# A fused linear-attention, capacity-routed expert and feed-forward kernel: the first search in pieces, and the first expert's second weights behind its rows

## What is computed

```python
# 1. gated linear attention: batch 4, 8 heads, 768 steps, head width 40
for t in range(S):
    m_new = max(f_gate + m, i_gate)
    C = exp(f_gate + m - m_new) * C + exp(i_gate - m_new) * outer(v, k)
    n = ... the same with k alone
    y[t] = sigmoid(o_gate) * (C @ q) / max(|n @ q|, 1)
x = y as 3072 rows of 320
# 2. routing: each token gets one of 8 experts, each expert 384 tokens
logits = x @ w_gate
for idx in argsort(-logits.flatten()):          # highest score first
    tok, e = idx // 8, idx % 8
    if not assigned[tok] and counts[e] < 384: assign tok to e
# 3. each expert
out[mask] = relu(x[mask] @ w1[e]) @ w2[e]       # 320 -> 1024 -> 320
# 4. on all rows
h = out @ w_in                                  # 320 -> 2048
result = (max(h, 0) + alpha * min(h, 0)) @ w_out
```

## Time and profile before

| | us |
|---|---|
| median of 3 runs | 823.14 (821.55 to 823.72) |
| the profiled execution | 826.35 |
| its span on the core | 824.6 |
| TensorE busy (share of the span) | 767.3 (93%) |
| VectorE busy | 585.4 (71%) |
| ScalarE busy | 323.3 (39%) |
| GpSimd busy | 166.5 (20%) |
| mean granted TensorE clock | 0.953 |

### The profile page before, as it was taken

The page is one execution under the profiler, slowest core; times in us unless marked ns, Lnnn a source line. Parts: engine busy times, 40 slices in busy tenths (PEclk is TensorE's granted clock), DMA queues, the critical chain, the costliest instruction groups (busy, mean ns, idle before and its releaser), DMA issues.

```text
span 824.6 us, 17035 instructions
## 1 busy us (share of the span) xinstructions
PE 767.3 (93%) x5535; PEld 719.1 (87%) x5535; DVE 585.4 (71%) x1454; ACT 323.3 (39%) x775; POOL 166.5 (20%) x244
## 2 busy tenths in 40 slices
PE   4999999984299999999999999999999999999995
PEld 3999999973188998899899889989998998999995
DVE  5766777766767886887787778768867886884442
ACT  4655666620213441452345135323613441352331
POOL 7356777510100011021001101100110110011001
PEclk9989999975589999999999999999999999999998
DMA  7787888510500410140041005003100400230000
GB/s 162 194 227 202 235 219 220 141 39 2 169 1 1 141 29 25 33 138 24 0 140 29 24 0 169 24 0 115 54 24 0 149 27 16 67 101 25 1 1 24
DMA packets 73407, 65.78 MB, mean 80 GB/s; under 512 B 35232, under 2 KB 64544, under 8 KB 73376
## 3 DMA queue, kind: packets, MB, share of 16 engines
q1 hardware_dynamic: 63584, 51.94, 22.7%
q0 software_dynamic: 2688, 8.65, 3.3%
q10 hardware_dynamic: 7104, 4.79, 1.8%
HBM read 56.71 MB, written 8.65 MB: 79 GB/s over the span
## 4 chain that ended last, share of the span: by engine, by line
PE 87%; DVE 8%; issue 2%; DMA 1%; ACT 1%; SPq 0%; POOL 0%; ACTq 0%; DVEq 0%
PE bank L825 19%; PE bank L827 17%; PE bank L826 17%; PE bank L668 6%; PE bank L715 5%; PE bank L843 4%; PE bank L844 4%; PE bank L703 2%; PE bank L696 2%; PE bank L679 2%; PE bank L749 1%; PE bank L660 1%; PE bank L868 1%; PE bank L869 1%; DMA s<-w 1%
## 5 line engine op out<-in xcount | busy, mean ns | idle before, releaser
L825 PE MATMUL bank<-wo_hi,h_hi 128*128 128x320 f32 x384 | 120.8, 315 | 0.0
L827 PE MATMUL bank<-wo_hi,h_lo 128*128 128x320 f32 x384 | 118.7, 309 | 0.0
L826 PE MATMUL bank<-wo_lo,h_hi 128*128 128x320 f32 x384 | 118.0, 307 | 0.0
L1484 DVE SCALAR_TENSOR_TENSOR g_act<-g_neg,rest_alpha,bank 128x384 f32<-128x384 f32 x128 | 78.6, 614 | 44.5 <-ACT g_neg L1058 43.5
L592 POOL DMA_INDIRECT xe<-x_rows,idx_in x24 | 24.4, 1015 | 407.0 <-DVE idx_in L1424 355.5
L1058 ACT ACTIVATE g_neg<-bank 128x384 f32<-128x384 f32 x128 | 62.8, 491 | 101.6 <-PE bank L844 101.6
L1056 ACT ACTIVATE h_hi<-bank 128x384 fp32r<-128x384 f32 x64 | 31.5, 491 | 170.4 <-PE bank L844 170.4
L1062 ACT CAST h_hi<-g_act 128x384 fp32r<-128x384 f32 x128 | 65.6, 512 | 79.5 <-DVE g_act L1484 79.0
L825 PE MATMUL bank<-yT_hi,wi_hi 128*128 128x384 f32 x256 | 92.3, 361 | 0.3 <-DVE yT_lo L1510 0.3
L827 PE MATMUL bank<-yT_hi,wi_lo 128*128 128x384 f32 x256 | 86.7, 339 | 0.0
L826 PE MATMUL bank<-yT_lo,wi_hi 128*128 128x384 f32 x256 | 86.7, 339 | 0.0
(11 more groups left out here) (229 smaller groups left out, 1834.2 us busy)
## 6 DMA issues: line engine op xcount, KB each, us to landing
s<-w SPq DMA_DIRECT2D x8, 1280.0 KB, 9.3
s<-w SPq DMA_DIRECT2D x8, 1024.0 KB, 5.2
s<-w SPq DMA_DIRECT2D x16, 256.0 KB, 6.2
k_in<-kT SPq DMA_DIRECT2D x24, 160.0 KB
q_wide<-qT SPq DMA_DIRECT2D x48, 80.0 KB
k_row<-k SPq DMA_DIRECT2D x24, 160.0 KB, 3.3
v_in<-v SPq DMA_DIRECT2D x24, 160.0 KB, 3.8
gate_o<-o SPq DMA_DIRECT2D x24, 160.0 KB, 3.0
```

What stands on the lines that cost most here:

```text
L825: pe.matmul(acc, ah, bh, start=start, stop=False, skip_group_check=True)
L826: pe.matmul(acc, ah, bl, start=False, stop=False, skip_group_check=True)
L827: return pe.matmul(acc, al, bh, start=False, stop=stop, skip_group_check=True)
L1484: dve.scalar_tensor_tensor(out=g_act[:, n, :], in0=g_neg[:, :], scalar=rest_alpha[:, j:j + 1], in1=acc, op0=ALU.mult, op1=ALU.add).then_in ...
```

## The change

- **Search.** `first_compare` works in three pieces of 10, 8 and 6 tiles (in the first step 20 and 4). The piece of 20 tiles is compared in `early_keys`, and `first_count` counts each piece as it comes; TensorE waits for the last logit's copy ahead of its first matmul. `first_flag` makes `flag` in one instruction with an accumulated output. Key values are scaled by 2^23, so that `keys_at_value` is one instruction.
- **Order of small steps.** In `make_keys` the maximum is taken and compared earlier, and three instructions are marked without a wait. The update of `route_value` goes from `take` to `reopen`; `closed_id` goes behind `member_sum`.
- **Rows.** `match_rows` makes each tile's one-hot rows with a `tensor_scalar` of 128 elements; `place_row` is now f32. This holds in all phases.
- **Weights.** In `load_weights` SP waits for `first_rows[1]` before it issues the first expert's second weights. ScalarE and VectorE take the rows before the second weights, whose last two thirds come behind `activate(0, 0)` and `split_hidden(0, 0)`.

Left out of the diff: `TOP`, `at_value` and `over_value` go, and `place_row` loses its BF16.

```diff
@@ -52,7 +52,8 @@
     assert REST == 64 and HB == 32 and CAP == 384 and S == NCH * P
-    VALUE_STEPS = [(5, 19), (5, 14), (5, 9), (5, 4), (4, 0)]
+    VALUE_AT = 23
+    VALUE_STEPS = [(5, VALUE_AT + 19), (5, VALUE_AT + 14), (5, VALUE_AT + 9), (5, VALUE_AT + 4), (4, VALUE_AT)]
     TIE_STEPS = [(5, 18), (5, 13), (5, 8), (5, 3)]
     STEPS = VALUE_STEPS + TIE_STEPS
     NS = len(STEPS)
...
@@ -352,6 +350,15 @@
             return slice(HB * (c % 4), HB * (c % 4) + HB)
+        def first_pieces(n):
+
+            ends = [0, NT - B, NT] if n == 0 else [0, 10, 18, NT]
+            return [slice(*pair) for pair in zip(ends, ends[1:])]
+
+        def pieces_before(n):
+
+            return sum(len(first_pieces(i)) for i in range(n))
+
         def bc(ap, n):
             return ap.unsqueeze(len(ap.shape)).to_broadcast(list(ap.shape) + [n])
@@ -455,6 +462,8 @@
                 sp.dma_start(s1[:, 0:2, :], w1[w, 0:2 * P, :].rearrange("(t p) f -> p t f", p=P)).then_inc(stage1_in, 16)
                 sp.dma_start(s1[0:REST, 2, :], w1[w, 2 * P:DM, :]).then_inc(stage1_in, 16)
                 sp.dma_start(s1[REST:P, 2, :], w1[w, 2 * P:DM, :]).then_inc(stage1_in, 16)
+                if first(e, 1):
+                    sp.wait_ge(first_rows[1], 16)
                 sp.dma_start(s2[:, :, :], w2[w].rearrange("(j p) d -> p j d", p=P)).then_inc(stage2_in, 16)
             load_weights(0)
@@ -752,9 +761,9 @@
             def first_count(n):
-                for half in range(2):
-                    pe.wait_ge(halves_ready, 2 * n + half + 1)
-                    for c in range(NT // 2 * half, NT // 2 * half + NT // 2):
+                for i, cs in enumerate(first_pieces(n)):
+                    pe.wait_ge(halves_ready, pieces_before(n) + i + 1)
+                    for c in range(cs.start, cs.stop):
                         ins = pe.matmul(CNT[0:JM, 0:E], above[:, JM * c:JM * c + JM], choice[:, c, :],
                                         start=(c == 0), stop=(c == NT - 1), skip_group_check=True)
                 ins.then_inc(count_ready, 1)
@@ -793,6 +802,7 @@
             pe.sem_inc(four_ready, NS)
+            pe.wait_ge(logit_read, NT)
             for n in range(NS):
                 first_count(n)
                 raise_base(0, n)
@@ -1041,8 +1051,6 @@
             for t in range(3):
                 high_w1(0, t)
-            for t in range(3):
-                high_w2(0, t)
             def rows_hi(e, t):
                 act.wait_ge(xe_turned, 3 * e + t + 1)
@@ -1083,7 +1091,10 @@
             for t in range(3):
                 rows_hi(0, t)
+            high_w2(0, 0)
             activate(0, 0)
+            high_w2(0, 1)
+            high_w2(0, 2)
             with act.Fori(0, E - 1) as e:
                 expert(e, True)
             expert(E - 1, False)
@@ -1169,12 +1180,15 @@
                 bits = logits[:, ts, :].bitcast(I32)
                 ch.link(dve.tensor_scalar(isign[:, ts, :], bits, 31, -2 ** 31, ALU.arith_shift_right, ALU.bitwise_or))
                 ch.link(dve.tensor_tensor(ibits[:, ts, :], bits, isign[:, ts, :], ALU.bitwise_xor))
-                ch.link(dve.tensor_scalar(isign[:, ts, :], ibits[:, ts, :], 8, None, ALU.logical_shift_right))
-                ch.mark(dve.tensor_copy(route_value[:, ts, :], isign[:, ts, :]))
+                ch.mark(dve.tensor_scalar(isign[:, ts, :], ibits[:, ts, :], 8, None, ALU.logical_shift_right))
                 ch.link(dve.tensor_scalar(ibits[:, ts, :], ibits[:, ts, :], 255, None, ALU.bitwise_and))
+                ch.mark(dve.tensor_scalar(route_value[:, ts, :], isign[:, ts, :], float(2 ** VALUE_AT), None, ALU.mult))
                 ch.link(dve.tensor_copy(tmp_a[:, ts, :], ibits[:, ts, :]))
+                ch.mark(dve.tensor_reduce(best_value[:, ts], route_value[:, ts, :], X, ALU.max))
                 ch.link(dve.scalar_tensor_tensor(out=route_tie[:, ts, :], in0=tmp_a[:, ts, :], scalar=float(2 ** 15), in1=route_tie[:, ts, :],
                                                  op0=ALU.mult, op1=ALU.add))
+                ch.link(dve.tensor_tensor(tmp_a[:, ts, :], route_value[:, ts, :], bc(best_value[:, ts], E), ALU.is_equal))
+                choose_tie(ch, ts)
             def choose_value(ch, ts):
@@ -1193,6 +1207,22 @@
                 choose_tie(ch, ts)
             KEY_LINKS = 15
+
+            def first_compare(n, pieces=None):
+
+                J = 2 ** STEPS[n][0] - 1
+                tie = n >= len(VALUE_STEPS)
+                key = key2 if tie else best_value
+                base = TIE_BASE if tie else VALUE_BASE
+                if n not in (0, len(VALUE_STEPS)):
+                    dve.wait_ge(base_ready, n)
+                for cs in pieces or first_pieces(n):
+                    st = steps[:, n, 0:J].unsqueeze(1).to_broadcast([P, cs.stop - cs.start, J])
+                    if n in (0, len(VALUE_STEPS)):
+                        dve.tensor_tensor(above_chunks(J)[:, cs, :], bc(key[:, cs], J), st, ALU.is_ge).then_inc(halves_ready, 1)
+                    else:
+                        dve.scalar_tensor_tensor(out=above_chunks(J)[:, cs, :], in0=bc(key[:, cs], J), scalar=base,
+                                                 in1=st, op0=ALU.subtract, op1=ALU.is_ge).then_inc(halves_ready, 1)
             def early_keys():
@@ -1202,7 +1232,7 @@
                 ch.mark(dve.memset(need[:, :], float(CAP)))
                 ch.mark(dve.memset(assigned[:, :, :], 0.0))
                 make_keys(ch, slice(0, NT - B))
-                choose(ch, slice(0, NT - B))
+                first_compare(0, first_pieces(0)[:1])
                 assert ch.n == KEY_LINKS, ch.n
             def make_probs(c, b):
@@ -1297,7 +1327,6 @@
             ch = Chain(dve, dve_step, STEP_LINKS * NT - B)
             dve.wait_ge(key_step, KEY_LINKS)
             make_keys(ch, slice(NT - B, NT))
-            choose(ch, slice(NT - B, NT))
             links0 = ch.base + ch.n
             def e_first(ap):
@@ -1307,7 +1336,7 @@
                 choose(ch, slice(0, NT))
-            LINKS = 27 + 2 * NS
+            LINKS = 25 + 2 * NS
@@ -1326,29 +1355,12 @@
                     dve.scalar_tensor_tensor(out=above_chunks(J), in0=bc(key[:, :], J), scalar=base,
                                              in1=st, op0=ALU.subtract, op1=ALU.is_ge).then_inc(above_ready, 1)
-            def first_compare(n):
-
-                J = 2 ** STEPS[n][0] - 1
-                tie = n >= len(VALUE_STEPS)
-                key = key2 if tie else best_value
-                base = TIE_BASE if tie else VALUE_BASE
-                if n not in (0, len(VALUE_STEPS)):
-                    dve.wait_ge(base_ready, n)
-                for half in range(2):
-                    cs = slice(NT // 2 * half, NT // 2 * half + NT // 2)
-                    st = steps[:, n, 0:J].unsqueeze(1).to_broadcast([P, NT // 2, J])
-                    if n in (0, len(VALUE_STEPS)):
-                        dve.tensor_tensor(above_chunks(J)[:, cs, :], bc(key[:, cs], J), st, ALU.is_ge).then_inc(halves_ready, 1)
-                    else:
-                        dve.scalar_tensor_tensor(out=above_chunks(J)[:, cs, :], in0=bc(key[:, cs], J), scalar=base,
-                                                 in1=st, op0=ALU.subtract, op1=ALU.is_ge).then_inc(halves_ready, 1)
-
             def first_flag(ch, n):
                 J = 2 ** STEPS[n][0] - 1
                 dve.wait_ge(count_ready, n + 1)
-                ch.link(dve.tensor_tensor(hit[0:J, :], CNT[0:J, 0:E], need[0:J, :], ALU.is_ge))
-                dve.tensor_reduce(flag[0:J, :], hit[0:J, :], X, ALU.max).then_inc(flag_ready, 1)
+                dve.tensor_scalar(hit[0:J, :], CNT[0:J, 0:E], float(CAP), 0.0, ALU.is_ge, ALU.max,
+                                  accum_out=flag[0:J, :]).then_inc(flag_ready, 1)
             def own_blocks(ch, ph, n):
@@ -1367,18 +1379,14 @@
             def keys_at_value(ch, ph):
                 dve.wait_ge(base_ready, ph * NS + len(VALUE_STEPS))
-                ch.mark(dve.scalar_tensor_tensor(out=at_value[:, :], in0=best_value[:, :], scalar=VALUE_BASE,
-                                                 in1=best_tie[:, :], op0=ALU.is_equal, op1=ALU.mult))
-                ch.link(dve.tensor_scalar(over_value[:, :], best_value[:, :], VALUE_BASE, TOP, ALU.is_gt, ALU.mult))
-                dve.tensor_tensor(key2[:, :], at_value[:, :], over_value[:, :], ALU.add).then_inc(keys_ready, 1)
+                dve.scalar_tensor_tensor(out=key2[:, :], in0=best_value[:, :], scalar=VALUE_BASE,
+                                         in1=best_tie[:, :], op0=ALU.subtract, op1=ALU.add).then_inc(keys_ready, 1)
                 dve.wait_ge(keys_ready, ph + 1)
             def take(ch, ph):
                 dve.wait_ge(base_ready, ph * NS + NS)
                 dve.scalar_tensor_tensor(out=taken[:, :, :], in0=bc(key2[:, :], E), scalar=TIE_BASE, in1=choice[:, :, :],
                                          op0=ALU.is_ge, op1=ALU.mult).then_inc(taken_ready, 1)
```

(24 more changed lines are left out.)

5 lines of the change are left out of this document (1 added, 4 removed).

## The result

The changed kernel takes 817.16 us in the median (814.53 to 818.41), against 823.14 (821.55 to 825.67) before: a ratio of 0.992, 95% interval 0.9896 to 0.9944, so 4.6 to 8.6 us faster. In the last experiment, with more executions on both sides, the same kernel gave 0.9908 (0.9885 to 0.993). The forecast was 4.05 us faster.

A forecast was written before the change was run, and what follows sets the result against it. TensorE bounds the kernel (87% of the chain), so gains come only where it idles. Hand-over with search gains -2.75 and loop -1.3 sum to -4.05, off the 823.14 us median: 819.1, range 816.6 to 821.8.

The forecast's parts named there:

- the three places: Where time could be won: first expert's search (185 to 218 us), hand-over to that expert (218 to 236), seven short loop waits.
- The loop: In seven experts, one-instruction `keys_at_value` removes TensorE's 0.2 us wait before the comparison with `key`: -1.3 us.
- The search: First expert's routing, all edits together: -2.1 us to the row indices, -2.3 to `order`, which releases the weights.
- The late keys and the first count: Last logit to first `hit`: two unwaited marks -0.26 us, late comparison of only 4 tiles -0.92.
- The flag: Search steps, `hit` to base matmul: one instruction with accumulated output saves 0.10 us in each of nine steps, -0.9.
- Rival (d): Search steps: the flag costs as much as before, +0.9 us, giving 820.0; chance 0.05.
- Rows by scalar: One-hot rows: 24 instructions of 128 elements at 0.155 us replace three of 1024, +0.3 us.
- Rival (a): One-hot rows: scalar instructions cost the full 1.05 ns an element, +2.3 us, giving 821.4; chance 0.12.
- The hand-over: First expert's start: first matmul 4.7 us earlier, second weights landing in 5.7 us, next search's count at 232.8, -2.75.
- (b): Hand-over: the second weights' transfer needs 9.3 us even alone, +3.6 us, giving 822.7; chance 0.08.
- (c): Hand-over: a 0.8 us pause before `down1(0)` delays TensorE's clock rise to 235.7, +1.4 us, giving 820.5; chance 0.09.
- (e): Hand-over: SP's gate makes it slower, gathers still 6.2 us, second weights landing at 233.8, +6.7, giving 825.8; chance 0.04.

The follow-up runs named there:

- the last experiment: The changed kernel run again unaltered, for its time and a second profile: 817.75 us, ratio 0.9908 to the kernel before.
- the experiment: The changed kernel with an unused tile of 192 bytes behind `key2`, moving all later tiles; run once: period of an expert 73.42 us against 73.32.
- the one kept busy: Changed kernel without SP's wait, old one-hot rows, second weights' first third ahead of rows, plus 18 unread matmuls keeping TensorE busy: ratio 0.9909.
- the gate on the first gather: The changed kernel with SP waiting for `first_rows[0]` instead of `first_rows[1]`; run once: count 25.08 us after SP's first weight issue against 22.82.

## Why the prediction was right or wrong

**What bounds the kernel: right**, with the three places it named; none of the difference lies elsewhere but the spread of the attention, which the forecast had in the profiled time only as the 3.2 us above the median.

**The loop: wrong in size, and this is the miss that counts.** The mechanism was right: `keys_at_value` stood ahead of the very comparison that TensorE waits for. The failed step is "more than the wait can't be won: -1.3", which took 0.20 us for the wait. The wait was 0.37, since the row counts from a matmul's shown end. That makes 0.36 x 7 = 2.5, where the sum had 1.3. Undoing the one edit brought the gap back to 0.54 from start to start (2.6 us in seven experts), and with what else came with it took the kernel back to a ratio of 0.9986. The remaining 0.9 of the loop's 3.46 was not in the sum: 0.07 an expert at `rank_members`, which the prediction priced for the first search and didn't carry over to the loop, and 0.06 in small parts, of which the tiles' places (0.10 for 192 bytes in the experiment) may be the cause; that part was not separated for this pair.

**The search: right, a little small.** -2.6 to `order`, forecast -2.3. The late keys and the first count met their sum (-1.19 against -1.18), three pieces gave 0.27 in eight steps against 0.3, the keys 0.37 against 0.37. The flag was the mis-sized term: 0.10 taken, 0.17 measured. It is indeed two instructions, as the Trainium skill (VectorE: DVE Perf Modes, "Two Vector instructions with no wait between them") says and the row `DVE_READ_ACCUMULATOR` shows, but the second is 0.07 us long and starts 0.09 behind the first, where 0.15 had been taken for it. `add_blocks` to the logit came out 0.2 larger than forecast, for TensorE at the slow clock held up `carried`, a limit the forecast did not see; in four other profiles the stretch is 10.34 to 10.35 us, +0.46, as forecast. Rival (d), a flag that costs as much as before, is out.

**Rows by scalar: right on the rate, a little short on the price.** Forecast 0.155 between starts, measured 3.99 for 24, 0.163 each: +0.49 instead of +0.3. Rival (a), full price an element, is out: that would be 0.254. With 0.034 us for the elements, as the forecast took them, the fixed part between starts is 0.13, where 0.12 had been taken.

**The hand-over: right in its course, wrong in its balance.** First matmul 4.5 us earlier from `add_blocks` (3.6 in the second profile; forecast 4.7), and what was late next was the second weights with VectorE behind them, as said. But they took 6.5 and 7.2 us from issue to use in the two profiles, and 6.3 to 6.7 in the six others with the gate in its place, where 5.7 had been taken and 6.1 was the upper end. From the first gather to the count it had been 16.8 us, the forecast had 16.1 (216.7 to 232.8), and it took 16.6 and 17.2. With the old order behind the new search it took 16.0, with the clock rising earlier by itself, and without the gate 16.1. So TensorE's early start came true and brought nothing at the count. The term that was mis-sized is the landing of the second weights, too short by 0.8 and 1.5 us in the two profiles. And the sum compared the new course with the old one at the old search's times; it never asked what the old hand-over would make of the new search, which is the same or a little better.

**The rivals.** (b) was the bound on the right side: not 9.3, but over 6.1. (c) didn't happen in the changed kernel: the clock rose at 224.7, 4.6 us after the first dense matmul, the pause of 1.03 us came after it, and the clock stayed. It is real in kind all the same: with the old rows a pause of 1.93 us at that place was followed by the low clock from 222.8 to about 226 us. Nor is 5.7 us a fixed delay: in these profiles, the one kept busy left out, the clock rose between 2.7 and 5.6 us after the first dense matmul. (e) is real in kind, and the gate on the first gather shows its mechanism: 2.3 us lost, with the gather at 7.2 us. In the changed kernel the weights start late enough to cost the third gather nothing in one profile and 0.5 us in the other.

**The sum.** -4.05 forecast; -5.86 between the profiles from `add_blocks` on and -5.98 between the medians; in the last experiment the medians lie 7.0 apart, so the near agreement of the first two is partly chance. Of the 1.8 missed, 2.2 are the loop, 0.3 the search up to `order`, and the hand-over takes 0.65 back. That the sum misses by less than the loop alone is luck.
